# Late tiles of an attention and mixture-of-experts kernel placed by float32r products of two parts, and four of them in place of three

## The chip, the cores and the metric

One core of a Trainium2 chip. The metric is the device time of the whole kernel in microseconds; one profiled execution gives the trace, in which all rows below stand.

## The reference, cut to what matters

```python
y = decay_attention(r, k, v, w, u)            # batch 2, 8 heads, 768 steps, head size 48
x = y.transpose(0, 2, 1, 3).reshape(1536, 384)
expert = argmax(x @ w_gate, axis=1)           # 8 experts, one for each token
slot = number_of_earlier_tokens_of(expert)    # a token is dropped from slot 384 on
h = relu(rows_of_expert @ w1[e])              # 384 -> 1024
y = gate * (h @ w2[e])                        # 1024 -> 384, back in the tokens' order
out = (layernorm(solu(y @ w_in)) * g_ln) @ w_out
```

The attention runs over time in order, so the tokens of the last tiles are known last. An expert's product can only begin when the places of its tokens are known.

## The kernel before, in words

The 1536 tokens are 12 tiles of 128 rows. A first loop (`for t in range(NT)`, on every engine) computes one tile a step; step t also finishes tile t-1: TensorE splits the turned rows (`split_x`, L1515), VectorE takes the gate logits (`take_logits`, L1051), ScalarE copies the rows to SBUF (`take_x`, L784). For groups of tiles (`GROUPS`) VectorE picks the experts (`pick_experts`, L1057 to L1080) one step after the group's last tile, TensorE counts the earlier tokens (`count_before`, L1531 to L1536) two steps after it, and VectorE makes the slots (`place_tokens`, L1087 to L1095). GpSimd scatters the rows of each tile to their slots in a DRAM buffer that is sorted by expert (`scatter`, L556).

SP loads the rows of expert 0 as soon as the tiles ahead of `LATE` are scattered (L461 to L462). For each late tile VectorE makes a 0/1 matrix `columns_of` (`late_columns`, L1105 to L1115) that has a one where a token belongs to a row of expert 0, and TensorE multiplies the tile's rows by it (`place_late`, L1541 to L1547), accumulating in three PSUM banks; `place_first_rows` (L1549 to L1557) adds the rows that came from DRAM and raises `xe_turned` for each bank. ScalarE then takes the rounded part (`act_first_xe_hi`, L698 to L702) and VectorE the remainder (`dve_first_xe_lo`, L939 to L944), and the eight expert passes begin (`pe_up`, `pe_down`), each product there a pair of float32r products (L1357 with 448 columns, L1358 with 224). GpSimd scatters the late tiles for the other experts once SP's load of the first rows has landed (L624 to L627).

The order of work is written out by hand, and each engine runs its own list in order. On ScalarE a step is: `take_y` of the tile before (L771), the odd diagonal (`put_diagonal`, L758), `take_x`, `take_k` (L765), the even diagonal of the next step, `gate_exp` (L790), and in the last two steps one part of expert 0's first weights (`act_w1_hi`, L708). After the loop come `take_last_y` (L779), more weight parts, `take_x` of tile 11 and `act_w2_hi` (L714). On VectorE a step begins with two masks (`mask_scores`, L1034), of which the second waits for the odd diagonal; in each step stands `add_own` (L1016), whose result the diagonals need; after the loop come the last picks and columns, two remainders of weights (`lo_w1`, L512) and the remainders of the first rows. `columns_of` lies in the buffer of the scores, and the first column waits for the output of step 10 (L1114).

## Time and profile before

| | us |
|---|---|
| median of 3 runs | 330.14 (329.66 to 330.14) |
| the profiled execution | 329.34 |
| its span in the trace | 327.6 |
| TensorE busy | 312.2 (95% of the span) |
| VectorE, ScalarE, GpSimd busy | 210.9, 196.1, 187.8 |
| first product of pass 0 | starts at 81.37 |

The profiled execution is 1.7 us longer than its span and 0.8 us shorter than the median. Times in rows count from the start of the span. A row of a timeline gives the start, the length and, in brackets, how long the engine was idle before it and what ended that. An engine's next instruction may start before the one before has ended, so what an instruction takes of its engine is read from start to start. PE is TensorE, PEld its weight load; DVE is VectorE, ACT ScalarE, POOL GpSimd, and SPq the DMA queue of SP.

### The profile page before, as it was taken

To read this page: it belongs to the slowest core of one execution; us is meant where nothing else is said; L and a number is where in the kernel's file an instruction comes from. 1 tells how busy PE (TensorE), PEld (TensorE's weight loads), DVE (VectorE), ACT (ScalarE), POOL (GpSimd) and SP (SyncE) were. 2 spreads that over 40 slices of the span, in tenths; PEclk is the share of its full clock that TensorE was granted. 3 is DMA by queue.
4 is the path that set the end of the run, shared out by engine and by line. 5 is a ranking of instruction groups with operands and counts; after the bars stand their busy time and mean duration, and the time that the engine had idled before them with its cause. 6 is when DMAs were issued, how large, how long until landed. Compare 5 with 4: busy or idle time off the path is not lost.

```text
span 327.6 us, 6566 instructions
## 1 busy us (share of the span) xinstructions
PE 312.2 (95%) x2378; PEld 281.5 (86%) x2380; DVE 210.9 (64%) x479; ACT 196.1 (60%) x374; POOL 187.8 (57%) x170
## 2 busy tenths in 40 slices
PE   7799999988999999999999999999999999999991
PEld 3588888877999999999999999788999999999991
DVE  7757757797765746555555556888987676655610
ACT  2478776877666767667675757456565544543520
POOL 5966678971699797989898969401031111111221
PEclk9999999999999999999999999999999999999997
DMA  8999999893597948575666684000010000000010
GB/s 139 156 285 267 240 244 263 215 392 121 187 399 255 319 146 285 184 246 196 232 202 228 229 270 177 5 1 2 1 50 8 16 26 24 24 26 25 26 47 26
DMA packets 62898, 50.65 MB, mean 155 GB/s; under 512 B 42512, under 2 KB 58256, under 8 KB 62864
## 3 DMA queue, kind: packets, MB, share of 16 engines
q1 hardware_dynamic: 59104, 45.25, 47.7%
q0 software_dynamic: 1920, 4.73, 3.9%
q10 hardware_dynamic: 1840, 0.21, 0.9%
q8 instruction: 21, 0.34, 0.5%
q14 instruction: 13, 0.11, 0.1%
HBM read 38.37 MB, written 11.82 MB: 153 GB/s over the span
## 4 chain that ended last, share of the span: by engine, by line
PE 83%; POOL 4%; issue 4%; DVE 3%; DMA 3%; ACT 1%; DVEq 0%; POOLq 0%; ACTq 0%; SPq 0%
PE ps L1357 25%; PE ps L1648 15%; PE ps L1631 15%; PE ps L1358 12%; PE ps L1657 3%; PE ps L1515 2%; PE ps L1493 2%; PE ps L1461 2%; PE ps L1430 2%; DMA rk_in<-in_k_dram 2%; DMA u_all<-in_u_dram 1%; PE ps L1351 1%; POOL own_place L567 1%; POOL own_place L571 1%; PE ps L1476 1%
## 5 line engine op out<-in xcount | busy, mean ns | idle before, releaser
L512 POOL TENSOR_TENSOR w_lo<-w_raw,w_hi 128x768 fp32r<-128x768 f32 x33 | 60.4, 1855 | 10.3 <-DVE w_lo L518 9.8
L1357 PE MATMUL ps<-xe,w_hi 128*128 128x448 f32 x192 | 61.8, 378 | 0.3
L1357 PE MATMUL ps<-h,w_hi 128*128 128x448 f32 x192 | 61.8, 378 | 0.0
L1648 PE MATMUL ps<-w_hi,h 128*128 128x384 f32 x192 | 51.6, 340 | 0.0
L1358 PE MATMUL ps<-h,w_lo 128*128 128x224 f32 x192 | 50.9, 265 | 0.0
L1358 PE MATMUL ps<-xe,w_lo 128*128 128x224 f32 x192 | 50.8, 264 | 0.0
L664 POOL TENSOR_TENSOR rstd<-var_b,minus_half 128x1 f32<-128x1 f32 x12 | 6.8, 565 | 72.4 <-DVE var_b L1303 72.4
L1631 PE MATMUL ps<-w_hi,xe 128*128 128x512 f32 x144 | 46.5, 393 | 0.7 <-ACT xe L876 0.7
L949 DVE TENSOR_TENSOR ps<-ps,rk_in 128x448 f32<-128x448 f32 x32 | 20.2, 632 | 32.7 <-ACT rk_in L718 32.7
L1357 PEld LDWEIGHTS ps<-xe,w_hi 128*128 128x128 f32 x192 | 36.0, 188 | 4.9 <-issue 2.1
L518 POOL TENSOR_TENSOR w_lo<-w_raw,w_hi 128x1024 fp32r<-128x1024 f32 x16 | 38.1, 2406 | 1.9 <-DVE w_lo L518 1.9
L1357 PEld LDWEIGHTS ps<-h,w_hi 128*128 128x128 f32 x192 | 36.1, 188 | 2.7 <-ACT h L725 0.2
L1358 PEld LDWEIGHTS ps<-h,w_lo 128*128 128x128 f32 x192 | 36.7, 191 | 0.0
L1358 PEld LDWEIGHTS ps<-xe,w_lo 128*128 128x128 f32 x192 | 36.7, 191 | 0.0
L1648 PEld LDWEIGHTS ps<-w_hi,h 128*128 128x128 f32 x192 | 35.0, 188 | 0.0
L1631 PEld LDWEIGHTS ps<-w_hi,xe 128*128 128x128 f32 x144 | 27.1, 188 | 6.6 <-issue 1.2
L758 ACT ACTIVATE scores<-ident,own 128x128 f32<-128x128 f32 x92 | 29.3, 390 | 5.6 <-DVE own L1016 4.9
L1648 PE MATMUL ps<-w_lo,h 128*128 128x384 f32 x96 | 32.2, 336 | 0.0
L714 ACT ACTIVATE w_hi<-w_raw 128x1024 fp32r<-128x1024 f32 x24 | 24.5, 1055 | 8.6 <-PE ps L1358 7.9
L708 ACT ACTIVATE w_hi<-w_raw 128x768 fp32r<-128x768 f32 x36 | 29.4, 839 | 0.0
L1631 PE MATMUL ps<-w_lo,xe 128*128 128x512 f32 x72 | 28.2, 392 | 0.0
L1274 DVE TENSOR_REDUCE hmax<-ps 128x1 f32<-128x512 f32 x24 | 16.1, 686 | 18.2 <-PE ps L1631 18.2
(166 smaller groups left out, 617.3 us busy)
## 6 DMA issues: line engine op xcount, KB each, us to landing
w_raw<-in_moe_w_dram SPq DMA_DIRECT2D x15, 1536.0 KB, 7.4
x_slots<-zeros SPq DMA_DIRECT2D x6, 768.0 KB, 5.9
rk_in<-in_r_dram SPq DMA_DIRECT2D x12, 192.0 KB, 5.6
rk_in<-in_k_dram SPq DMA_DIRECT2D x12, 192.0 KB, 6.0
v_in<-in_v_dram SPq DMA_DIRECT2D x12, 192.0 KB, 5.5
out_dram<-zeros SPq DMA_DIRECT2D x1, 2304.0 KB, 8.1
w_raw<-in_moe_w_dram SPq DMA_DIRECT2D x3, 512.0 KB, 5.4
rows_in<-x_slots SPq DMA_DIRECT2D x8, 192.0 KB, 7.8
```

The source lines that it names most:

```text
L512: eng.tensor_tensor(w1_lo[:, :, cols], w1_raw[:, i, :, cols], w1_hi[:, :, cols].bitcast(F32), ALU.subtract).then_inc(g.w1_lo, 1)
L518: eng.tensor_tensor(w2_lo[:, :, cols], w2_raw[:, i, :, cols], w2_hi[:, :, cols].bitcast(F32), ALU.subtract).then_inc(g.w2_lo if d == 0 els ...
L708: act.activation(w1_hi[:, :, cols], w1_raw[:, i, :, cols], ACT.Copy).then_inc(hi_sem, 1)
L714: act.activation(w2_hi[:, :, cols], w2_raw[:, i, :, cols], ACT.Copy).then_inc(hi_sem, 1)
L758: last = act.activation(scores[:, t % 2, a, p, :], ident[:], ACT.Copy, scale=own[:, 2 * p + a:2 * p + a + 1])
L949: dve.tensor_tensor(first_sums(j, g.n), first_sums(j, g.n), h_rest[:, j % 2, :, 0:g.n], ALU.add)\
L1274: dve.tensor_reduce(hmax[:, a:a + 1], hidden_banks(t)[:, a, :], AX_X, ALU.max).then_inc(max_step, 1)
L1357: pe.matmul(ps[:, bank, 0:2 * n], w_hi, x[:, c, 0:2 * n], start=first, stop=False, skip_group_check=True)
L1358: return pe.matmul(ps[:, bank, 0:n], w_lo, x[:, c, 0:n], start=False, stop=last, skip_group_check=True)
L1631: last = pe.matmul(hidden_banks(t)[:, a, :], xt[:, c, i * P:(i + 1) * P], wt[:, c, a * 512:(a + 1) * 512], start=(c == 0 and z == 0), stop ...
L1648: last = pe.matmul(ps[:, OB + i, 0:DM], ht[:, f, i * P:(i + 1) * P], wt[:, f, :], start=(f == 0 and z == 0), stop=(f == KF - 1 and z == 2))
L1657: last = pe.transpose(ps[:, TB + f // 4, (f % 4) * P:(f % 4 + 1) * P], solu[i][:, f * P:(f + 1) * P], ident[:])
```

## The change

`LATE` gets a fourth tile, tile 8, and the group of tiles 6 to 8 becomes one of tiles 6 and 7 and one of tile 8 alone. For each late tile ScalarE writes the rows once more, rounded to float32r (`late_hi`), and GpSimd writes the remainder; TensorE places both by two float32r products where one float32 product stood. Both, and the columns, lie in the buffer `h` of the hidden layer, and the first column no longer waits for an output of the loop. The first late column is made within step 10, the last late tile is placed behind the first rows, and `xe_turned` is raised there. SP's load of the first rows waits for 8 scattered tiles in place of 9.

```diff
--- before.py
+++ after.py
@@ -143,8 +143,10 @@
 
 
 
-        LATE = [NT - 3, NT - 2, NT - 1]
-        columns_of = scores[:, 0].rearrange("p a h t -> p (a h t)")[:, 0:3 * N1].rearrange("p (t n) -> p t n", t=3)
+        LATE = [NT - 4, NT - 3, NT - 2, NT - 1]
+        h_place = h[:].rearrange("p f n -> p (f n)")
+        late_x = h_place[:, 0:2 * len(LATE) * DM].rearrange("p (t z d) -> p t z d", t=len(LATE), z=2)
+        columns_of = h_place[:, 2 * len(LATE) * DM:2 * len(LATE) * DM + len(LATE) * N1].rearrange("p (t n) -> p t n", t=len(LATE))
         column_key = rows_in[:, 1].rearrange("p m d -> p (m d)")[:, 0:N1]
         column_key_i = rows_in[:, 0].rearrange("p m d -> p (m d)")[:, 0:N1].bitcast(I32)
 
@@ -198,7 +200,7 @@
         EVEN_PAIRS = [h for h in range(H) if h // 2 % 2 == 0]
         ODD_PAIRS = [h for h in range(H) if h // 2 % 2 == 1]
         TOT = slice(CNT + 128, CNT + 128 + E)
-        GROUPS = [range(0, 3), range(3, 6), range(6, 9), range(9, 10), range(10, 11), range(11, 12)]
+        GROUPS = [range(0, 3), range(3, 6), range(6, 8), range(8, 9), range(9, 10), range(10, 11), range(11, 12)]
 
         HB, OB, TB = 0, 4, 6
         XA, XC = 2, 3
@@ -301,6 +303,8 @@
         first_odd_ready = sem("first_odd_ready")
         key_ready = sem("key_ready")
         columns_ready = sem("columns_ready")
+        late_x_hi = sem("late_x_hi")
+        late_x_lo = sem("late_x_lo")
         late_rank = sem("late_rank")
         late_slot_a = sem("late_slot_a")
         late_slot_b = sem("late_slot_b")
@@ -614,13 +618,17 @@
                             pool.wait_ge(picked_ready, n + 1)
                     own_parts(t + 1)
                 for _ in range(2):
-                    if t >= GROUPS[group_of(stored)][-1] + 4:
+                    if stored < LATE[0] and t >= GROUPS[group_of(stored)][-1] + 4:
                         if stored == 0:
                             pool.wait_ge(slots_zeroed, 16 * ZERO_PARTS)
                         scatter(stored)
                         stored += 1
             for t in range(stored, LATE[0]):
                 scatter(t)
+            for j in range(len(LATE)):
+                pool.wait_ge(late_x_hi, j + 1)
+                pool.tensor_tensor(late_x[:, j, 1], x_rows(LATE[j]), late_x[:, j, 0].bitcast(F32), ALU.subtract)\
+                    .then_inc(late_x_lo, 1)
             for m in range(usual.tiles):
                 pool.wait_ge(usual.rows_loaded[0][m], 16)
             for t in LATE:
@@ -784,6 +792,10 @@
                 act.activation(x_rows(t).rearrange("p (q n) -> p q n", q=HP), pairs_of_x()[:, :, 0:2 * D], ACT.Copy)\
                     .then_inc(x_ready, 1)
 
+            def late_hi(j):
+                act.wait_ge(x_ready, LATE[j] + 1)
+                act.activation(late_x[:, j, 0], x_rows(LATE[j]), ACT.Copy).then_inc(late_x_hi, 1)
+
             def gate_exp(n):
                 g = GROUPS[n]
                 act.wait_ge(below_ready, n + 1)
@@ -806,12 +818,15 @@
                 for n, g in enumerate(GROUPS):
                     if t == g[-1] + 2:
                         gate_exp(n)
+                if t - 1 in LATE:
+                    late_hi(LATE.index(t - 1))
                 if t >= NT - 2:
                     act_w1_hi(act, 0, usual.w1_in[0], w1_loads(0, 1), usual.w1_hi, parts=[t - NT + 2])
             take_last_y()
             gate_exp(len(GROUPS) - 2)
             act_w1_hi(act, 0, usual.w1_in[0], w1_loads(0, 1), usual.w1_hi, parts=[2])
             take_x(NT - 1)
+            late_hi(len(LATE) - 1)
             act_w1_hi(act, 0, usual.w1_in[0], w1_loads(0, 1), usual.w1_hi, parts=[3])
             gate_exp(len(GROUPS) - 1)
             act_w2_hi(act, 0, usual.w2_in[0], 16, usual.w2_hi, parts=[0, 1])
@@ -1111,7 +1126,6 @@
                 dve.wait_ge(late_slot_a, j + 1)
                 if j == 0:
                     dve.wait_ge(key_ready, 2)
-                    dve.wait_ge(y_done, NT - 1)
                 dve.tensor_scalar(columns_of[:, j], column_key, slot_a[:, t:t + 1], None, ALU.is_equal).then_inc(columns_ready, 1)
 
             def late_slots():
@@ -1156,14 +1170,16 @@
                         else:
                             place_tokens(n)
                         add_picked(n)
-            late_columns(0)
-            rank_late(1)
+                        if g[-1] == LATE[0]:
+                            late_columns(0)
+            late_columns(1)
+            rank_late(2)
             add_picked(len(GROUPS) - 2)
             take_logits(NT - 1)
             pick_experts(len(GROUPS) - 1)
-            late_columns(1)
-            rank_late(2)
             late_columns(2)
+            rank_late(3)
+            late_columns(3)
             late_slots()
             add_picked(len(GROUPS) - 1)
 
@@ -1541,10 +1557,13 @@
             def place_late(j):
 
                 pe.wait_ge(columns_ready, j + 1)
-                pe.wait_ge(x_ready, LATE[j] + 1)
+                pe.wait_ge(late_x_lo, j + 1)
                 for c in range(KD):
-                    pe.matmul(first_turned(c), x_rows(LATE[j])[:, c * P:(c + 1) * P], columns_of[:, j],
-                              start=(j == 0), stop=False, skip_group_check=True)
+                    for z in range(2):
+                        last = pe.matmul(first_turned(c), late_x[:, j, z, c * P:(c + 1) * P], columns_of[:, j],
+                                         start=(j == 0 and z == 0), stop=(j == len(LATE) - 1 and z == 1), skip_group_check=True)
+                    if j == len(LATE) - 1:
+                        last.then_inc(usual.xe_turned, 1)
 
             def place_first_rows():
 
@@ -1552,9 +1571,8 @@
                     pe.wait_ge(usual.rows_loaded[0][m], 16)
                 for c in range(KD):
                     for m, rows in enumerate(usual.rows):
-                        last = pe.matmul(first_turned(c)[:, m * P:m * P + rows], rows_in[0:rows, 0, m, c * P:(c + 1) * P],
-                                         ident[0:rows, 0:rows], start=False, stop=(m == 1), skip_group_check=True)
-                    last.then_inc(usual.xe_turned, 1)
+                        pe.matmul(first_turned(c)[:, m * P:m * P + rows], rows_in[0:rows, 0, m, c * P:(c + 1) * P],
+                                  ident[0:rows, 0:rows], start=False, stop=False, skip_group_check=True)
 
             pe.wait_ge(zero_ready, 1)
             keep_warm(10, UB)
@@ -1583,10 +1601,11 @@
             count_before(len(GROUPS) - 2)
             split_x(NT - 1)
             place_late(0)
+            place_late(1)
             count_before(len(GROUPS) - 1)
-            place_late(1)
             place_late(2)
             place_first_rows()
+            place_late(3)
             pe.wait_ge(sum_ready, len(GROUPS))
             pe.wait_ge(late_rank, len(LATE))
             pe.matmul(ps[:, UB, TOT], ones_bf[:], picked_sum[:], start=True, stop=True).then_inc(total_done, 1)
```

## Rows read from the trace of the kernel before

**Rows 1.** Windows: us; busy us (x instructions) per engine; granted clock; DMA share; GB/s
```profile
68.44:75.19 6.75, 5.18 (x70) 4.45 (x69) 5.93 (x26) 5.87 (x17) 3.59 (x5) 1.00 1.02 407
75.19:81.37 6.18, 5.61 (x35) 4.84 (x35) 4.90 (x19) 4.04 (x9) 0.97 (x1) 1.00 0.20 70
...
81.37:210.00 128.63, 127.85 (x814) 119.66 (x815) 76.61 (x130) 85.48 (x136) 111.93 (x63) 1.00 0.65 226
```

**Rows 2.** Chain of waits: start us, us, what; around the last late tiles
```profile
74.22 1.15 PE ps L1515 x8
...
76.74 0.35 DVE scores L1115
...
77.13 2.54 PE ps L1546 x12
...
79.75 1.55 PE ps L1555 x12
```

**Rows 3.** Timeline of ScalarE, step 9 to the first rows: start us, us, instruction
```profile
63.68 0.57 ACT L771 ACTIVATE yt<-ps 128x512 f32<-128x512 f32 x1
...
66.63 0.49 ACT L784 ACTIVATE w_raw<-ps 128x384 f32<-128x384 f32 x1 [1.20 <-DVE logits L1051]
67.01 0.59 ACT L765 ACTIVATE place<-ps 128x512 f32<-128x512 f32 x1
...
69.11 0.21 ACT L790 ACTIVATE lexp<-below 128x24 f32<-128x24 f32 x1
69.22 0.83 ACT L708 ACTIVATE w_hi<-w_raw 128x768 fp32r<-128x768 f32 x1
69.96 0.57 ACT L771 ACTIVATE yt<-ps 128x512 f32<-128x512 f32 x1
...
72.58 0.49 ACT L784 ACTIVATE w_raw<-ps 128x384 f32<-128x384 f32 x1 [0.88 <-DVE logits L1051]
...
80.44 1.25 ACT L702 ACTIVATE xe<-ps 128x224 fp32r<-128x224 f32 x3 [1.61 <-PE ps L1555]
```

**Rows 4.** Timeline of TensorE: the splits of tiles 9 and 10
```profile
64.72 1.14 PE L1515 MATMUL ps<-pick_pair,yt 128*128 128x104 f32 x8
...
70.58 1.14 PE L1515 MATMUL ps<-pick_pair,yt 128*128 128x104 f32 x8 [0.98 <-ACT yt L771]
```

**Rows 5.** Timeline of TensorE: neighbouring float32r products in pass 0
```profile
84.74 0.26 PE L1358 MATMUL ps<-xe,w_lo 128*128 128x224 f32 x1
84.84 0.38 PE L1357 MATMUL ps<-xe,w_hi 128*128 128x448 f32 x1
85.05 0.26 PE L1358 MATMUL ps<-xe,w_lo 128*128 128x224 f32 x1
```

**Rows 6.** Timeline of VectorE: outliers, weight remainders, remainders of the first rows
```profile
63.23 1.50 DVE L1080 TENSOR_TENSOR picked<-lscore,top 128x24 bf16<-128x24 f32 x1
...
68.55 0.60 DVE L1095 SCALAR_TENSOR_TENSOR slot<-slot_a,slot_b 128x3 int32<-128x3 f32 x1
...
78.37 1.82 DVE L512 TENSOR_TENSOR w_lo<-w_raw,w_hi 128x768 fp32r<-128x768 f32 x2
80.83 1.29 DVE L943 TENSOR_TENSOR xe<-ps,xe 128x224 fp32r<-128x224 f32 x3 [0.64 <-ACT xe L702]
```

**Rows 7.** GpSimd: costliest groups on the page, then its timeline
```profile
L512 POOL TENSOR_TENSOR w_lo<-w_raw,w_hi 128x768 fp32r<-128x768 f32 x33 | 60.4, 1855 | 10.3 <-DVE w_lo L518 9.8
...
72.01 0.97 POOL L556 DMA_INDIRECT x_slots<-w_raw,slot  x1 [0.30 <-issue]
80.38 0.97 POOL L556 DMA_INDIRECT x_slots<-w_raw,slot  x1 [7.40 <-DMA rows_in<-x_slots]
```

**Rows 8.** SP's queue, then DMA issues with us to landing
```profile
77.08 0.81 SPq L457 DMA_DIRECT2D rows_in<-x_slots  x2
...
rows_in<-x_slots SPq DMA_DIRECT2D x1, 192.0 KB, 2.2
...
meta<-token,sorted_to POOLq DMA_INDIRECT x12, 6.4
```

## The prediction

> **What bounds the kernel now.** I read the stages first [rows 1]. From 81.37 us on, TensorE is busy 127.85 of 128.63 us: the expert passes are bound by TensorE, and the change edits nothing in them. So it can only move the moment at which the first product of pass 0 starts, 81.37 us, and everything behind that moment keeps its distance to it. Ahead of it lie two stretches in which TensorE is not full: 68.44 to 75.19 (5.18 busy of 6.75) and 75.19 to 81.37 (5.61 of 6.18), all at a granted clock of 1.00, the 2.4 GHz level.
>
> The chain of waits says what those two stretches hang on [rows 2]: the split of the last chunk on TensorE (L1515, 74.22), the last tile's logits and picks on VectorE, the column of a late tile (L1115, 76.74), then two placements (L1546, 77.13, 2.54 us) and the first rows (L1555, 79.75, 1.55 us). Last I read the engines' own timelines, because ScalarE stands ahead of this chain: its rows from 69.11 to 69.96 are back to back [rows 3], and before the split of tile 10 TensorE sat idle 0.98 us for ScalarE's L771 [rows 4].
>
> **The change, part by part.**
>
> *Placement on TensorE.* Before, a late tile is three float32 products; the trace records two MATMULs for each, so 12 records are two tiles: 2.54 / 2 = 1.27 us a tile [rows 2]. After, it is six float32r products of 224 columns, each with its own weight load. The nearest row is a float32r product of the same 224 columns, L1358: 84.74 to the start of its successor at 84.84, 0.10 us [rows 5]. There a 448-column neighbour may cover the load, so the upper bound is the product of the first rows, the narrowest with a load of its own: 1.55 / 12 = 0.129 us [rows 2]. I take 0.11: 0.66 us a tile (bounds 0.60 and 0.77), 0.61 less than now. The Trainium skill ("TensorE: Matmul & The Clock Gate", LDWEIGHTS) gives a load as columns / 1.2, 107 ns for 128; by that estimate a tile is 0.64 us, the two results being 0.02 us apart.
>
> Four tiles cost 4 x 0.66 = 2.64 against 3.81 us, but two of the four (8 and 9) go ahead of the last count, where TensorE waits for picks anyway. On the path stood 2.54 (two tiles) + 1.55, with the first `xe_turned` after a third of the rows: 2.54 + 0.08 + 0.52 = 3.14 us after 77.13, and ScalarE's L702 starts at 80.44 [rows 3]. After, it is one tile, all rows, and a third of the last tile: 0.66 + 1.55 + 0.22 = 2.43. Gain at `xe_turned`: 0.7 us.
>
> *What that gain runs into.* VectorE must first end the two weight remainders that start at 78.37 and last 1.82 us (to 80.19), and its L943 then sat idle 0.64 us [rows 6]. These precede the remainders of the first rows in VectorE's order and stay there. So of the 0.7 us at most 0.64 can be had; ScalarE was idle 1.61 us before L702 and takes tile 11's new copy within that.
>
> *ScalarE's four new copies* (`late_hi`, 128x384, SBUF to float32r). The nearest row is L784, the same 384 elements: 66.63 to the next start at 67.01, 0.38 us of the engine [rows 3]; L708 with 768 elements goes 69.22 to 69.96, 0.74, so half of it is 0.37 and no less. One more group also adds a `gate_exp`, 69.11 to 69.22, 0.11. Three copies stand in the loop, each *ahead of* the next `take_y` and `put_diagonal`:
> - Step 9: `gate_exp` and tile 8's copy push `take_y(9)` from 63.68 to 64.17. TensorE's split of tile 9 starts at 64.72 and needs it at 64.17 + 0.57 = 64.74: no loss. The split's row is in [rows 4]. But the odd diagonal, the second mask, the logits and `take_x(9)` (66.63) all go 0.49 later. The diagonal after it also waits for VectorE's `own`, which depends on GpSimd and moves less; I take 0.11 as regained (bounds 0 and 0.49). Shift 0.38.
> - Step 10: tile 9's copy stands ahead of `act_w1_hi` part 0 and `take_y(10)`: 69.96 becomes 70.72. Shift 0.76. This is the wait that shows as 0.98 us before L1515; it grows. The odd diagonal comes right behind it, and the mask that waits for that diagonal and the logits follow.
> - Step 11: `take_x(10)` (72.58), then tile 10's copy, then part 1 of the weights, then L779. Shift 1.14.
>
> So the split of tile 11 starts at 74.22 + 1.14 = 75.36, and the picks, columns and weight remainders on VectorE behind it go 1.14 later too. The Trainium skill ("ScalarE: Activation LUTs", What ACT_TABLE_LOAD costs) gives an ACTIVATE with immediates 186 ns + 0.833 ns an element and 93 ns of overlap back to back: an estimate of 0.41 us a copy, which makes the shift 1.14 + 3 x 0.03 = 1.23. Its 506 ns for one agrees with the 0.49 us of the row; the overlap is what differs.
>
> The trace's 0.38 stands in my sum.
>
> *VectorE.* Step 8 gains the pick of tiles 6 and 7; step 9 gets their placing, an `add_picked` and one single-tile pick in place of a pick of three tiles, some ten operations of about 0.2 us where five were; step 10 loses about as much and gains a column. That delays the first mask of step 10, but the second one waits for the odd diagonal anyway; cost 0, and up to 1.3 us if an outlier like the 1.50 us L1080 at 63.23 or the 0.60 us L1095 at 68.55 falls there, where the copies of such size take about 0.2 [rows 6]. After the loop its work is what it was: the fourth column is made within step 10.
>
> *GpSimd.* Four subtractions of 128x384, half of L512's 1.855 us for 768 elements each, 0.93 us [rows 7]. They stand between the early scatters and a wait that was 7.40 us long. The fourth waits for tile 11's copy, which ends some 2.3 us after the split that starts at 75.36 (split 1.15, logits 0.2, `take_x` and copy 0.49 each), near 77.7, and so ends near 78.6; its product is due about 80.5. Cost 0. Behind them in its queue stand the late scatters, four instead of three, each 0.97 + 0.30 us: from 79.7 they end near 84.8, and a weight part of 1.86 us after them ends at 86.7. Its product is the 19th pair of pass 0, which at 0.31 us a pair (84.74 to 85.05 [rows 5]) comes near 87.5. Cost 0, with 0.8 us of cover. SP's loads for pass 1 wait for these scatters too and go out some 0.8 us later; they are wanted a whole pass on. Cost 0.
>
> *SP's load of the first rows.* It waits for the scatters ahead of the late tiles: 9 before, 8 after. The last one started at 72.01 [rows 7] and the load was issued at 77.08, 5.07 us later, landing 2.2 us after issue [rows 8]. Tile 7's scatter starts one scatter (1.27) and the old wait for slots (0.3) earlier, near 70.4: by 5.07, loads at 75.5, both landed at 75.5 + 0.43 + 2.2 = 78.1. Wanted: 77.13 + 1.14 + 0.66 = 78.93. Cost 0; cover 0.8 us.
>
> *Sum.* By TensorE: 77.13 + 1.14 + 2.43 = 80.70 for `xe_turned`, against 80.27; ScalarE + 0.43. By VectorE: 80.19 + 1.14 = 81.33 for its first remainder, against 80.83: + 0.50. VectorE ends last, so pass 0 starts at 81.87 and the span is 0.50 us longer. The profiled execution, 329.34 us, becomes 329.84. The median of the runs shown is 330.14, 0.8 above the profiled one, so for the median I give 330.14 + 0.5 = 330.6. A measurement of this kernel can tell about 0.2% (0.66 us) from no change: 0.5 us is within it.
>
> **Rivals.**
> 1. *The first rows come late* (slower). Tile 7's scatter lies wholly in the stretch where the DMA engines are full (407 GB/s, against 70 behind 75.19) [rows 1], tile 8's had the drained end; the scatters of tokens landed after 6.4 us [rows 8]. By 6.4 us the loads go out at 76.8, land at 79.4, 0.5 us too late, and the products of rows and of the last tile stand behind them in TensorE's order: + 0.95 us, 331.1. It decides from a landing over 78.9 on. If the scatter gains nothing at all and rows land at 79.7, + 1.3, 331.4. Against it: a head start of 1.3 us or more. Chance 0.2.
> 2. *ScalarE's idle time takes the copies.* It was idle 1.20 and 0.88 us before its two L784 in the trace [rows 3]. If the copies of tiles 8 and 9 vanish there, the shift is 0.38 and VectorE's 0.64 of idle outweighs it: -0.26, 329.9; with none left, -0.64, 329.5. Against it: each copy stands behind the wait, not in it, ahead of work that the next step wants. Chance 0.15.
> 3. *VectorE becomes the bound in steps 9 and 10*, by stretched small operations of the new group: + 0.5 to + 1.3 beyond my sum, 331.1 to 331.9. For it: 63.23 and 68.55. Chance 0.1.
> 4. *The placement is not cheaper* (0.21 us for each product, as each record of L1546 takes now): a tile stays at 1.27 us, the path is 1.27 + 1.55 + 0.42 = 3.24 against 3.14, and with the shift pass 0 starts 1.24 us later, 331.4. The 0.10 us of L1358 speaks against it. Chance 0.03.
>
> **How the numbers follow.** My own case, shift of 0.9 to 1.3 us and VectorE last, gives + 0.3 to + 0.7, 330.4 to 330.8: chance 0.5; it reaches 0.2% only at its top. 0.02 is left for what I don't see. The range takes rival 2 to its -0.64 and rivals 1 and 3 up to + 1.5: 329.5 to 331.7. Faster by over 0.2% needs more than the whole 0.64 of VectorE's idle time: 0.07. Slower by over 0.2%: rivals 1, 3 and 4 (0.33) and a little of my own case: 0.38. Within: 0.55.
>
> **What would show it.** Right: L1546 at about 0.11 us a record; ScalarE's copies of 0.49 us directly ahead of L771; the wait before the split of tile 10 grown from 0.98 to about 1.4 us; the last split at 75.3; no idle time on VectorE before L943; pass 0 starting at 81.9; the stages behind it unchanged. Wrong: TensorE idle before the first rows with a DMA as releaser (rival 1); the last split still at 74.3 (rival 2); a late mask in step 10 or 11 with VectorE busy before it (rival 3). A change of the passes' own length would overturn the frame.

## The result and the profile after

The kernel after takes 332.75 us (median of 20 executions, 330.43 to 334.78), the kernel before, beside it, 329.61 us (20 executions, 328.35 to 330.41): a ratio of 1.008 [1.0061, 1.01], so the change makes it slower by 0.8%. The profiled execution of after took 331.01 us with a span of 329.2: 1.67 us more than the profiled execution of before. The prediction, 330.6 us and no measurable difference as the likeliest case, was wrong, and 332.75 lies above its range.

Two things have to be explained: the 1.67 us that the profiled executions differ by, and why the median of 20 executions lies another 1.7 us above the profiled one. For the first, the windows of after: step 10 of the loop, and then the stretches of [rows 1], cut at the same events (the columns are those of [rows 1]):

```profile
63.44:69.58 6.14, 5.92 (x84) 4.99 (x82) 5.96 (x17) 4.49 (x14) 5.75 (x7) 1.00 1.01 350
69.58:76.95 7.37, 5.13 (x70) 4.39 (x69) 6.00 (x23) 6.49 (x18) 5.20 (x6) 1.00 0.82 326
76.95:83.21 6.26, 4.97 (x43) 4.42 (x42) 5.65 (x19) 4.81 (x11) 2.34 (x3) 1.00 0.17 58
83.21:211.84 128.63, 127.77 (x816) 119.50 (x816) 76.80 (x130) 85.28 (x135) 112.78 (x64) 1.00 0.66 228
```

The expert passes are what they were, 128.63 us in both, and what follows them is 0.2 us shorter. Pass 0 starts at 83.21 in place of 81.37, 1.84 us later, and all of it arises ahead of it. TensorE's timeline says where:

```profile
63.44 1.71 PE L1477 MATMUL ps<-place 64*128 64x128 f32 x16
65.69 1.14 PE L1531 MATMUL ps<-pick_pair,yt 128*128 128x104 f32 x8
...
69.58 1.16 PE L1477 MATMUL ps<-place 64*128 64x128 f32 x16
71.94 1.14 PE L1531 MATMUL ps<-pick_pair,yt 128*128 128x104 f32 x8 [1.19 <-ACT yt L779]
...
76.04 1.14 PE L1531 MATMUL ps<-pick_pair,yt 128*128 128x104 f32 x8 [0.60 <-ACT yt L787]
76.95 1.58 PE L1563 MATMUL ps<-h 128*128 128x224 f32 x12
...
79.75 0.93 PE L1563 MATMUL ps<-h 128*128 128x224 f32 x6 [0.98 <-DVE h L1129]
80.52 1.48 PE L1574 MATMUL ps<-ident,rows_in 128*128 128x128 f32 x12
81.78 0.91 PE L1563 MATMUL ps<-h 128*128 128x224 f32 x6
...
83.21 0.44 PE L1373 MATMUL ps<-xe,w_hi 128*128 128x448 f32 x1 [0.27 <-ACT xe L710]
```

The first product of a step (L1477; L1461 before) and the splits (L1531; L1515 before) can be laid beside those of before:

| start, us | step 10 | step 11 | split of tile 10 | split of tile 11 | pass 0 |
|---|---|---|---|---|---|
| before | 63.01 | 68.44 | 70.58 | 74.22 | 81.37 |
| after | 63.44 | 69.58 | 71.94 | 76.04 | 83.21 |
| later by | 0.43 | 1.14 | 1.36 | 1.82 | 1.84 |

Of the 0.43 us, 0.38 is there at step 8 already (52.85 against 52.47), where no edited instruction has run; the runs below start their step 8 between 52.47 and 53.84, so this much is an offset of the execution. (The three latest, 53.56 to 53.84 in `a1_same`, `g2_all` and `f2_three_warm`, are the traces in which the granted clock was 0.50 from about 16 to 19 us, far ahead of anything that was edited; all others start it at 52.91 or sooner.) The change itself costs 1.46 us: 0.05 in step 9, 0.71 in step 10 (6.14 us long against 5.43), 0.68 from the start of step 11 to the last split, and 0.02 behind it, where 0.64 us was to be won.

ScalarE, the copies (L797) and what stands behind them (beside [rows 3]):

```profile
70.16 0.51 ACT L797 ACTIVATE h<-w_raw 128x384 fp32r<-128x384 f32 x1
70.57 0.83 ACT L716 ACTIVATE w_hi<-w_raw 128x768 fp32r<-128x768 f32 x1
71.31 0.58 ACT L779 ACTIVATE yt<-ps 128x512 f32<-128x512 f32 x1
...
74.46 0.52 ACT L797 ACTIVATE h<-w_raw 128x384 fp32r<-128x384 f32 x1
74.89 0.83 ACT L716 ACTIVATE w_hi<-w_raw 128x768 fp32r<-128x768 f32 x1
75.62 0.64 ACT L787 ACTIVATE yt<-ps 128x256 f32<-128x256 f32 x2
```

A copy takes 0.41 and 0.43 us of ScalarE from start to start (0.38 was expected; tile 11's, from 77.96 to 78.40, takes 0.44), and the two splits wait 1.19 us in place of 0.98 and 0.60 in place of 0.15 for exactly the work behind it.

GpSimd and VectorE are the surprise (beside [rows 6, 7]). First GpSimd, then VectorE:

```profile
64.19 1.02 POOL L583 TENSOR_TENSOR place<-rk_in,wlast 128x384 f32<-128x384 f32 x1
...
75.06 0.99 POOL L630 TENSOR_TENSOR h<-w_raw,h 128x384 fp32r<-128x384 f32 x1 [0.80 <-ACT h L797]
78.57 1.00 POOL L630 TENSOR_TENSOR h<-w_raw,h 128x384 fp32r<-128x384 f32 x1 [2.51 <-ACT h L797]
```

```profile
63.70 1.55 DVE L1076 SCALAR_TENSOR_TENSOR lscore<-logits,lmax,desc 128x8 f32<-128x8 f32 x1
...
65.48 0.34 DVE L1081 TENSOR_SCALAR picked<-lscore,top 128x8 bf16<-128x8 f32 x1
...
65.87 1.52 DVE L1049 COPY_PREDICATED scores<-causal,ps 128x512 f32<-128x512 int32 x2
...
75.22 0.97 DVE L1129 TENSOR_SCALAR h<-rows_in,slot_a 128x224 fp32r<-128x224 f32 x1
...
78.56 1.14 DVE L1129 TENSOR_SCALAR h<-rows_in,slot_a 128x224 fp32r<-128x224 f32 x1
...
80.01 0.34 DVE L1129 TENSOR_SCALAR h<-rows_in,slot_a 128x224 fp32r<-128x224 f32 x1
...
80.88 1.81 DVE L516 TENSOR_TENSOR w_lo<-w_raw,w_hi 128x768 fp32r<-128x768 f32 x2
82.67 0.99 DVE L958 TENSOR_TENSOR xe<-ps,xe 128x224 fp32r<-128x224 f32 x3
```

The same column (L1129) takes 0.34 us with GpSimd idle and 0.97 and 1.14 us beside a remainder on GpSimd. Each long one ends with the GpSimd instruction: 78.56 + 1.14 = 79.70 against 78.57 + 1.00 = 79.57; 75.22 + 0.97 = 76.19 against 76.05; and 63.70 + 1.55 = 65.25 against 64.19 + 1.02 = 65.21. I call this a hold. The masks (L1049, one operand from PSUM) aren't held: two take 1.52 us beside GpSimd and took as much before. The outliers of [rows 6] are holds too: 63.23 + 1.50 = 64.73, while a GpSimd product ran from 63.66 to 64.68. The Trainium skill ("SBUF — State Buffer", SBUF: two separate sides) names a port pair that VectorE and GpSimd share as an exclusive lock, taken by whichever starts first, among others where a VectorE instruction has two SBUF inputs and the GpSimd one reads SBUF. The lengths agree with it, even for an instruction of 128x8 elements. Who goes first can't be read from the recorded starts: VectorE's is the earlier one, by 0.01 us at 78.56, by 0.49 at 63.70 and by 0.43 in the row of before at 63.23, and yet VectorE was held.

The wait of 0.98 us at 79.75 is such a hold. Last, TensorE's timeline prices the placement: from 79.75 to 80.52 a tile takes 0.77 us, not 0.66.

### The profile page after: what moved, and what is told of

It reads as the page before. It is cut to its first block, busy times and chain, and to the rows that moved or that the text cites. A ratio compares the mean times of both kernels' runs of the same rounds, so it can differ in the third digit from the quotient of the medians.

```text
span 329.2 us, 6608 instructions
## 1 busy us (share of the span) xinstructions
PE 312.5 (95%) x2387; PEld 281.7 (86%) x2387; DVE 214.6 (65%) x489; ACT 198.1 (60%) x379; POOL 192.3 (58%) x174
## 4 chain that ended last, share of the span: by engine, by line
PE 86%; ACT 4%; DVE 3%; issue 2%; POOL 1%; DMA 1%; DVEq 0%; SPq 0%; POOLq 0%; ACTq 0%
PE ps L1373 25%; PE ps L1667 15%; PE ps L1650 15%; PE ps L1374 12%; PE ps L1509 4%; PE ps L1676 3%; PE ps L1531 3%; PE ps L1477 3%; PE ps L1446 2%; ACT scores L766 2%; PE ps L1504 1%; PE ps L1492 1%; PE ps L1367 1%; DMA wsq<-in_w_dram 1%; DVE place L977 1%
```

## The experiments

Twelve runs in three groups, each group with runs of the kernel before on the same chip: 31 executions with a median of 330.58 us for the a-kernels; 25, 329.91 us, for b, c and f1; 33, 330.2 us, for g, f2 and h1. Each group stands under its texts of expectation, which name theories: **L**, VectorE's instructions are held by GpSimd's remainders; **C**, ScalarE's copies ahead of `take_y` cost; **D**, the pick of the new group's tile 8 delays step 10; **G**, idle time lets TensorE's granted clock fall in some executions; **N**, nothing but noise.

### The change again, the copies and the holds

`a1_same` is the kernel after, unchanged.

> The changed kernel once more, unchanged, beside the others. Its 20 executions lie in two heaps, near 331.1 and near 333.5 us, and the granted clock of a whole execution is 0.99 in most of the first and 0.98 in most of the second. Theory G (TensorE's clock falls to its lower level in some executions): such an execution shows a stretch with a granted clock below 1.00 after one of the waits ahead of pass 0, and is 2 to 3 us longer. Theory N (only noise in the loads): the clock is 1.00 everywhere up to the end and the spread comes from the loop. Both expect a ratio of 1.006 to 1.010.

332.04 us, ratio 1.0048 [1.0022, 1.0075]. Slower again, by less. Its trace has the same holds of the columns (0.97 and 1.14 us) and a last split 6.32 us into step 11 (6.46 in after), but its step 10 takes 5.73 us where that of after took 6.14, with the same code: a single trace can be off by 0.4 us there. Between 50 and 90 us its granted clock is 1.00, so this trace shows nothing for theory G; two of the 12 executions have a mean clock under 0.988.

`a2_waits` lets each GpSimd remainder wait until VectorE's columns are made:

```diff
                 pool.wait_ge(late_x_hi, j + 1)
+                pool.wait_ge(columns_ready, [1, 2, 2, 4][j])
```

> GpSimd's remainder of tile 8 waits for the first column, those of tiles 9 and 10 for the second, that of tile 11 for the fourth, so that no column is written while a remainder runs. Theory L (VectorE's column from two SBUF operands is held while GpSimd's remainder runs): L1129 takes 0.34 us each of the last three times instead of 0.97, 1.14 and 0.34, the third column is ready 0.8 us earlier, and pass 0 starts 0.7 to 0.8 us earlier than in the changed kernel; 0.7 us off the time in the faster heap. Theory C alone (only the copies on ScalarE cost): the columns keep their lengths, no gain.

332.19 us, 1.0041 [1.0019, 1.0064]. The holds of the columns are gone and nothing is won. VectorE's timeline says why:

```profile
78.43 0.34 DVE L1130 TENSOR_SCALAR h<-rows_in,slot_a 128x224 fp32r<-128x224 f32 x1
...
79.87 0.98 DVE L1136 SCALAR_TENSOR_TENSOR slot<-slot_a,slot_b 128x4 int32<-128x4 f32 x1
...
81.01 1.81 DVE L516 TENSOR_TENSOR w_lo<-w_raw,w_hi 128x768 fp32r<-128x768 f32 x2
```

The last remainder now runs from 79.83 to 80.83 and holds the slots: 0.98 us where 0.16 is usual. TensorE is done with its last tile at 81.7, 0.8 us earlier than in after, and then waits 1.38 us for VectorE, whose weight remainders start at 81.01 against 80.88. A hold that is moved is still a hold, and behind the last column VectorE is the one that counts.

`a3_later` takes the copies out from ahead of `take_y` (tile 10's stands before the last `take_x`); `a4_both` is this and the wait of `a2_waits`:

```diff
             put_diagonal(t, 1)
+                if t - 2 in LATE:
+                    late_hi(LATE.index(t - 2))
...
-                if t - 1 in LATE:
-                    late_hi(LATE.index(t - 1))
...
+            late_hi(len(LATE) - 2)
```

> The copies of tiles 8, 9 and 10 go on ScalarE behind the odd diagonal of the next step, ahead of a wait for the logits of 0.9 to 1.2 us, tile 10's ahead of the last take_x. Theory C (they cost because they stand ahead of take_y): the last split of TensorE starts 1.1 us earlier than in the changed kernel, pass 0 starts 0.5 to 1.1 us earlier. Theory L alone: the remainders of GpSimd start later and still meet the columns, gain below 0.3 us. Theory G: if the wait before the split of tile 10 is what lets the clock fall, the slower heap is gone and the median falls by over 2 us.

> Both edits together. Theories C and L together: pass 0 starts 1.5 to 1.9 us earlier than in the changed kernel, at about 81.3, and the time is that of the kernel before or up to 0.6 us less (ratio 0.998 to 1.001). If one of the two is wrong, half of it.

332.96 us, 1.0056 [1.0028, 1.0083], and 332.03 us, 1.0043 [1.002, 1.0067]. From the start of step 11 to the last split takes 5.73 and 5.45 us, against 6.46 in after and 5.78 before: C holds, the copies cost those 0.68 us. But pass 0 starts at 83.69 and 83.16, where about 81.3 was expected of `a4_both`. Of the 83.69, 0.7 us are lost in steps 8 and 9, which take 5.53 and 5.74 us in this trace (5.27 and 5.32 in after), though the edit leaves step 8 alone and takes a copy out of step 9. The rest is in VectorE's timeline of `a3_later`:

```profile
77.61 0.87 DVE L1077 SCALAR_TENSOR_TENSOR lscore<-logits,lmax,desc 128x8 f32<-128x8 f32 x1
...
78.70 0.85 DVE L1082 TENSOR_SCALAR picked<-lscore,top 128x8 bf16<-128x8 f32 x1
```

Two remainders of GpSimd (77.43 to 79.53) now meet the last pick and hold two of its instructions, 0.64 and 0.62 us over the 0.23 us that each takes otherwise. In `a4_both` VectorE's weight remainders are the end, as in `a2_waits`: the last pick (0.98 us at 76.80) and the slots (0.98 us at 79.76) are held there. The four ratios of this group can't be told apart; what each edit does is read from the traces.

### The parts alone

`c1_nolo` has no remainders on GpSimd. It leaves that part of the computation out: TensorE multiplies the rounded part twice, so its work stays the same.

```diff
-            for j in range(len(LATE)):
-                pool.wait_ge(late_x_hi, j + 1)
-                pool.tensor_tensor(late_x[:, j, 1], x_rows(LATE[j]), late_x[:, j, 0].bitcast(F32), ALU.subtract)\
-                    .then_inc(late_x_lo, 1)
```

> GpSimd's four remainders are left out (a part of the computation: each late row goes in by its rounded part twice, so TensorE's work is the same). Theory L (GpSimd's remainders hold VectorE's operations on two or one SBUF operands): the second and third column take 0.34 us each instead of 0.97 and 1.14, VectorE starts its last two weight remainders 0.9 us earlier, and pass 0 starts 0.8 to 1.0 us earlier than in the changed kernel; what stays against the kernel before is about 0.5 to 1.0 us. Theory C alone: less than 0.2 us off.

331.04 us, 1.0038 [1.0015, 1.006]. The columns behind the loop:

```profile
74.85 0.34 DVE L1125 TENSOR_SCALAR h<-rows_in,slot_a 128x224 fp32r<-128x224 f32 x1
...
78.86 0.34 DVE L1125 TENSOR_SCALAR h<-rows_in,slot_a 128x224 fp32r<-128x224 f32 x1
```

Both take 0.34 us, and so does the last. The column of step 10, at 68.95 beside GpSimd's products of the keys, is held as in after (0.80 us; 0.73 there). L is shown: take the GpSimd instruction away and the hold goes. Pass 0 starts at 82.76, 0.45 us earlier than in after, where 0.8 to 1.0 was expected. The trace says what took the difference; first its windows, then TensorE's timeline:

```profile
72.00:74.00 2.00, 1.73 (x29) 1.50 (x29) 1.37 (x8) 1.12 (x5) 0.07 (x1) 0.92 1.02 397
74.00:76.00 2.00, 2.00 (x19) 1.63 (x16) 1.21 (x8) 1.99 (x7) 0.00 (x0) 0.50 0.26 101
```

```profile
71.59 1.14 PE L1527 MATMUL ps<-pick_pair,yt 128*128 128x104 f32 x8 [1.19 <-ACT yt L775]
...
75.68 1.80 PE L1527 MATMUL ps<-pick_pair,yt 128*128 128x104 f32 x8
```

The granted clock is 0.50, the 1.2 GHz level, from about 74 to 77 us, 2 us behind a wait of 1.19 us, the very wait that after has before its split of tile 10. The last split takes 1.57 us to the next start in place of 0.91, which is 0.66 us; with the 0.45 that makes 1.1 us, an estimate of what the kernel without remainders gains at an unchanged clock. Against the kernel before, some 0.7 us are left without any remainder.

`b2_nosplit` keeps the new groups and the four late tiles, but places them by the old float32 product: no copies, no remainders, the columns in a buffer of their own (`late_columns_place`).

```diff
-                    for z in range(2):
-                        last = pe.matmul(first_turned(c), late_x[:, j, z, c * P:(c + 1) * P], columns_of[:, j],
-                                         start=(j == 0 and z == 0), stop=(j == len(LATE) - 1 and z == 1), skip_group_check=True)
+                    last = pe.matmul(first_turned(c), x_rows(LATE[j])[:, c * P:(c + 1) * P], late_columns_place[:, j],
+                                     start=(j == 0), stop=(j == len(LATE) - 1), skip_group_check=True)
```

> The fourth late tile and the new groups alone, with one float32 product for each as before (no copies, no remainders). Theory D: the steps from the start of step 10 to that of step 11 take 5.9 to 6.3 us as in the changed kernel, against 5.43 before. Theories C and L alone: 5.5 us, and the last split starts no later than before by more than 0.2 us. Two float32 tiles of 1.27 us stand ahead of the last count, so pass 0 starts 1.0 to 1.5 us later than before whichever holds: ratio 1.003 to 1.006.

330.66 us, 1.0021 [1.0006, 1.0035], below the 1.003 to 1.006 that was expected, though pass 0 starts at 82.63, 1.26 us later than before, as expected. Step 10 takes 5.95 us against 5.43 before, with no copy in the kernel: this is D. All traces together bear it out: step 10 takes 5.73 to 6.30 us in the eight with the new group picked behind the placing (after, `a1_same` to `a4_both`, `b2_nosplit`, `c1_nolo`, `f1_warm`), and 5.36 to 5.68 in the four with the old groups (before, `b1_three`, `f2_three_warm`, `h1_best`). What happens can be read in the rows of after above. In both kernels an instruction of the pick is held until GpSimd's product of the keys ends, 1.67 us after the start of step 10 before and 1.77 us in after. Before, the held one was the last of the pick (L1080, [rows 6]), and the masks started at 64.65 (start to start an overlap of 0.08 us). After, placing tiles 6 and 7 stands ahead of the pick, the held one is its second (L1076), and L1079 to L1083 follow, so the masks start at 65.87: 2.43 us into the step, against 1.64. Their results feed the new state (L1062), and TensorE's count waits for that. Behind the loop the split of tile 11 starts 5.57 us into step 11, 0.21 less than before.

`b1_three` is the split alone: three late tiles and the old groups, with copies and remainders.

```diff
-        LATE = [NT - 4, NT - 3, NT - 2, NT - 1]
+        LATE = [NT - 3, NT - 2, NT - 1]
-        GROUPS = [range(0, 3), range(3, 6), range(6, 8), range(8, 9), range(9, 10), range(10, 11), range(11, 12)]
+        GROUPS = [range(0, 3), range(3, 6), range(6, 9), range(9, 10), range(10, 11), range(11, 12)]
```

> The split alone: three late tiles and the groups of before. Theory C+L: the last split of TensorE starts 0.8 us later than before (two copies in the loop), columns and picks are held by the remainders of tiles 10 and 11, ratio to before 1.002 to 1.004, and no loss in step 9 to 10. Theory D (the new group in step 9 is what costs): ratio within 1.000 to 1.001.

333.16 us, 1.0099 [1.0068, 1.0129] of 6 executions, where 1.002 to 1.004 was expected: worse than the whole change. Step 10 is back at 5.47 us, which bears out D from the other side. What it lost is in the windows and TensorE's timeline:

```profile
77.00:78.00 1.00, 0.33 (x3) 0.14 (x2) 0.89 (x6) 0.97 (x3) 0.00 (x0) 1.00 0.00 0
78.00:79.00 1.00, 0.19 (x2) 0.13 (x2) 0.97 (x1) 1.00 (x3) 0.97 (x1) 0.84 0.86 277
79.00:85.00 6.00, 5.79 (x27) 5.61 (x28) 3.70 (x12) 2.68 (x6) 3.11 (x4) 0.50 0.20 80
85.00:86.00 1.00, 1.00 (x6) 0.94 (x6) 0.90 (x6) 1.00 (x2) 0.00 (x0) 0.74 0.48 197
```

```profile
78.05 0.17 PE L1545 MATMUL ps<-picked,tri_bf 128*128 128x8 bf16 x1 [0.72 <-DVE picked L1081]
...
79.22 1.62 PE L1561 MATMUL ps<-h 128*128 128x224 f32 x6 [0.97 <-DVE h L1129]
80.64 2.74 PE L1572 MATMUL ps<-ident,rows_in 128*128 128x128 f32 x12
83.08 1.60 PE L1561 MATMUL ps<-h 128*128 128x224 f32 x6
```

From 79 to 85 us the granted clock is 0.50, the 1.2 GHz level, and the products of the first rows take 2.74 us in place of 1.48. In the two windows ahead of it TensorE was busy 0.33 and 0.19 of 1 us, in the second because its column (78.03, 1.13 us) was held. The Trainium skill ("TensorE: Matmul & The Clock Gate", What's actually happening) describes a clock that falls after idle time of the engine; the trace agrees in kind, and what stands ahead of the fall are waits of 1.26, 0.72 and 0.97 us with work between them.

This can be seen in the times of all executions, since each has its mean granted clock. Six us at half clock lower the mean over 330 us by 6 x 0.5 / 330 = 0.009, from about 0.993 to 0.984. The executions with a mean under 0.988:

| kernel | under 0.988 | kernel | under 0.988 |
|---|---|---|---|
| before, 89 beside the runs below | 3 | c1_nolo | 1 of 12 |
| after | 7 of 20 | b2_nosplit | 0 of 12 |
| a1_same | 2 of 12 | g1_pickfirst | 2 of 10 |
| a2_waits | 1 of 10 | g2_all | 3 of 12 |
| a3_later | 5 of 10 | h1_best | 1 of 12 |
| a4_both | 1 of 12 | f1_warm | 0 of 8 |
| b1_three | 5 of 6 | f2_three_warm | 0 of 12 |

The count is a lower bound and a rough one: the stretch of 3 us in `c1_nolo` leaves a mean of 0.991, and the early one at 16 us, which has nothing to do with the change, leaves 0.990 in `a1_same` and 0.989 in `f2_three_warm`. Nor is a low mean always a long time: the five of `a3_later` have a median of 332.58 us, the other five 332.96.

The 7 of after have a median of 333.56 us, the other 13 of 331.35, which is 1.74 above before's 329.61, as in the traces (1.67).

`f1_warm` puts products of zeros (`keep_warm`, about 0.25 us each) where TensorE of after waits: four ahead of the split of tile 10, two ahead of the last, four ahead of the tile that waits for the held column.

```diff
+                if t == NT - 1:
+                    keep_warm(4, RT)
...
+            keep_warm(2, RT)
...
+                keep_warm(4, RT)
             place_late(2)
```

> The changed kernel with ten products of zeros for TensorE in its three waits of 1.19, 0.60 and 0.98 us (4, 2 and 4 of some 0.22 us each). Theory G (executions with a mean clock below 0.988 are the ones in which TensorE's idle time lets the clock fall): none below 0.988, against 7 of 20 and 2 of 12 of the changed kernel and none of 31 of the kernel before, and no execution above 333 us on this chip's scale. If the clock falls for another reason the share stays near a quarter. The best executions are not faster than without (0 to +0.2 us).

331.21 us, 1.0036 [1.0018, 1.0055]. None of its 8 executions is under 0.988. Pass 0 starts at 82.87, as far behind step 8 as in after (30.40 us against 30.36).

### Repairs

`g1_pickfirst` picks tile 8 ahead of the placing of tiles 6 and 7.

```diff
+                if t == LATE[0] + 1:
+                    pick_experts(group_of(LATE[0]))
...
-                    if t == g[-1] + 1:
+                    if t == g[-1] + 1 and g[-1] != LATE[0]:
```

> The changed kernel, with tile 8 picked ahead of the placing of tiles 6 and 7 in step 9, so that the pick no longer meets GpSimd's product for the next keys. Theory D (the pick of the new group is held there for 1.3 us and delays step 10): the 1.5 us operation in step 9 is gone, the start of step 10 to that of step 11 takes 5.4 to 5.6 us instead of 6.14, pass 0 starts 0.5 us earlier than in the changed kernel. If the stall has another cause (TensorE itself paused in step 10 of the changed kernel), it stays at 5.9 or more.

331.55 us, 1.0052 [1.0034, 1.007]. The 1.5 us instruction is gone. Step 10 takes 5.70 us (5.4 to 5.6 was expected) against 6.14 in after; but `a1_same`, which doesn't have this edit, shows 5.73, so what the order is worth isn't shown by this run. The wait before the split of tile 10 grew, 1.50 against 1.19 us, since it hangs on ScalarE, and pass 0 starts at 83.27, where about 82.7 was expected.

`g2_all` adds to this the copies moved as in `a3_later` (tile 10's right behind `take_last_y`) and the remainders on VectorE:

```diff
-                pool.tensor_tensor(late_x[:, j, 1], x_rows(LATE[j]), late_x[:, j, 0].bitcast(F32), ALU.subtract)\
+                dve.tensor_tensor(late_x[:, j, 1], x_rows(LATE[j]), late_x[:, j, 0].bitcast(F32), ALU.subtract)\
```

> All three causes taken away from the changed kernel: the pick order of g1, ScalarE's copies in its idle time (tile 10's right behind the last take_y), and the remainders on VectorE (tile 8's in step 11, 9's and 10's before the last logits, 11's behind the last column) instead of GpSimd. Theories C, L and D together: no held operation above 0.5 us beside the two first steps, pass 0 starts at 81.4 to 82.0, ratio 0.999 to 1.002. If one of them is wrong, ratio 1.003 or more.

331.54 us, 1.005 [1.003, 1.007], where 0.999 to 1.002 was expected. Step 10 takes 5.30 us, less than before. Its profiled execution has a mean clock of 0.978 (the early stretch at 16 us is in it too) and shows the fall once more, in its windows, 2 us behind a wait of 1.35 us that ended at 71.97:

```profile
73.00:74.00 1.00, 0.74 (x19) 0.47 (x17) 1.00 (x3) 0.50 (x2) 0.00 (x0) 0.92 1.05 407
74.00:80.00 6.00, 5.68 (x35) 5.38 (x36) 4.62 (x25) 4.66 (x11) 0.00 (x0) 0.50 0.31 111
```

The clock doesn't account for the miss: its nine executions that aren't under 0.988 have a median of 331.31 us, still 1.1 above before. Taking L, C and D away doesn't repair the kernel with four late tiles. In its trace the remainders, 0.5 us each, now stand on VectorE's own path: one ahead of the second mask of step 11, for which TensorE waits 0.59 us (0.27 in after), and one behind the last column, so that the weight remainders start 6.49 us behind the last split (4.84 in after) and TensorE waits 1.34 us for VectorE before pass 0. Some of these 6.49 us are the lower clock; how much isn't shown.

`f2_three_warm` is `b1_three` with the products of zeros: four ahead of the split of tile 10, two ahead of the last count of the loop, two ahead of the last split, five ahead of the tile of the held column.

```diff
+                if t == NT - 1:
+                    keep_warm(4, RT)
...
+            keep_warm(2, RT)
...
+            keep_warm(2, RT)
+            keep_warm(5, RT)
```

> b1_three (three late tiles, split; five of its six executions had a mean clock below 0.988 and its trace a stretch at 0.50 from 79 to 85 us) with 13 products of zeros in TensorE's waits. Theory G: no execution below 0.988, the time 2.0 to 2.5 us less than b1's 333.2, ratio 1.002 to 1.004. If the lower clock is not from the idle time, the ratio stays near 1.010.

331.6 us, 1.0043 [1.0023, 1.0063], against 1.0099 [1.0068, 1.0129] without them: the intervals don't meet, and none of 12 executions is under 0.988 where 5 of 6 were. Nothing else in the kernel differs; the two ran on different chips, each with the kernel before beside it. G is shown for this kernel, and it is worth about 0.56% there. The holds and copies are still in it, and with them the other 0.4%.

`h1_best` takes the causes away rather than their effects: three late tiles and the old groups, the copies in ScalarE's waits, the remainders on VectorE, one weight remainder of VectorE's behind those of the first rows, and one load of weights on SP behind the load of the first rows. As a diff to `b1_three`, shortened:

```diff
-            load_w1(1, 1)
...
+            load_w1(1, 1)
...
+            late_lo(0)
+            late_lo(1)
...
+            late_lo(2)
...
-            lo_w1(dve, 0, 0, usual, parts=[1, 2])
+            lo_w1(dve, 0, 0, usual, parts=[1])
...
+            lo_w1(dve, 0, 0, usual, parts=[2])
```

> A version that might beat both: the groups and three late tiles of before, placed by split products; copies on ScalarE in its idle time, remainders on VectorE, VectorE's third weight remainder moved behind the first rows' remainders, and SP's load of expert 1's first weights (1536 KB) issued behind the load of the first rows so that the scatters land earlier. If theories C, L and D are right and nothing else binds: the last split as early as before, the first rows loaded before 77, pass 0 starts 0.6 to 1.0 us earlier than before, ratio 0.996 to 0.999. If the scatters' landing does not depend on that load, the first rows still come at 79.7 and the ratio is 1.000.

329.93 us against 330.2, 0.9993 [0.9972, 1.0015]: as fast as before, not faster. TensorE's timeline:

```profile
77.96 0.93 PE L1567 MATMUL ps<-h 128*128 128x224 f32 x6 [0.17 <-DVE h L1126]
78.72 1.48 PE L1578 MATMUL ps<-ident,rows_in 128*128 128x128 f32 x12
79.99 0.91 PE L1567 MATMUL ps<-h 128*128 128x224 f32 x6
...
81.41 0.44 PE L1377 MATMUL ps<-xe,w_hi 128*128 128x448 f32 x1 [0.49 <-ACT xe L706]
```

The last split starts at 74.92, 5.55 us into step 11 (6.46 in after), no column is held, and pass 0 starts at 81.41 against 81.37; counted from step 8 (52.83 and 52.47) that is 0.32 us earlier, where 0.6 to 1.0 was expected. SP's load of the first rows is issued at 75.23, 2.54 us behind the start of the scatter that it waits for (72.69), against 5.07 us before: from 70 to 72 us the busy share of the DMA engines is 0.18, where it is 1.03 in before with the load of weights still under way. The run makes several edits at once, and what each is worth isn't shown. No version that ran beats the kernel before by more than can be measured.

## Why the prediction was wrong

**What the prediction got right.** The expert passes didn't change. ScalarE's copies shift the last split, though by luck the size looks better than it is: 1.14 us were predicted for them, and the split moved by 1.44 (the offset of 0.38 taken off), but only the 0.68 us of step 11 are theirs. In step 9 next to nothing was lost (0.05 us), and of the 0.71 us of step 10 VectorE's part is 0.5, by `b2_nosplit`. The wait before the split of tile 10 grew (1.4 predicted, 1.19 measured). VectorE has no idle time before the remainders of the first rows, so its 0.64 us were used up as said. SP's load of the first rows was not the bound, though the reason given was wrong: it was issued at 77.10, as before (77.08, [rows 8]), and not at 75.5, though the scatter that it waits for started at 71.30, 0.7 us earlier. This is the second case of rival 1, rows at 79.7 (77.10 + 0.43 + 2.2), and `h1_best` speaks for its reason, the full DMA engines. TensorE reached the rows 1.6 us later than was reckoned, at 80.52 against 78.93, and that hid it: luck, and not a cover of 0.8 us.

**The step that failed: "GpSimd. [...] Cost 0".** The prediction counted when GpSimd would be done and who waits for its results. It didn't ask what VectorE can do while GpSimd works. The last remainder (1.00 us long, 0.93 reckoned) held the third column for 0.80 us (1.14 against 0.34), on the path of both engines: TensorE waited 0.98 us for that column, and VectorE's weight remainders start 2.51 us later than before (80.88 against 78.37), of which 1.82 are the late split and 0.69 came behind it. Evidence: the ends of the rows coincide, `c1_nolo` removes it, `a2_waits` and `a3_later` move it onto other instructions of VectorE.

**"VectorE. [...] cost 0, and up to 1.3 us if an outlier [...] falls there"** is the same error seen from the other side. The 1.50 us at 63.23 was no outlier: a GpSimd product ended 0.05 us before it. The sum had seen that the new group delays the first mask and let the second one's wait for the odd diagonal hide it. In the trace both masks ran one behind the other with no wait, 0.79 us late in the step, and the count of step 10 waited for what they feed. That is rival 3 with its mechanism, and 0.5 us of step 10's 0.71 by `b2_nosplit` (5.95 against 5.43). Rival 3 reached up to 331.9 in the prediction's own words, and the range, which ended at 331.7, cut it off.

**The sum, put right.** Predicted: 1.14 - 0.64 = +0.50 us. Measured in the profiled execution, by VectorE: offset 0.38, shift 1.44, hold 0.69, less 0.64 of VectorE's idle time: 1.87 us. By TensorE and ScalarE: offset 0.38, shift 1.44, hold 0.80, less the 0.78 us by which the way from the placement behind the column to pass 0 is shorter (79.75 to 83.21 against 77.13 to 81.37): 1.84 us, and pass 0 does start 1.84 us later, with ScalarE as the one it waited for. So both ways end within 0.03 us of each other, and taking the hold off one of them alone, as in `a2_waits`, wins nothing.

**Mis-sized terms.** The placement takes 0.77 us a tile, the upper bound that was given, not 0.66: L1358 with 0.10 us stands between products of 448 columns, which may cover its load (no run takes that apart), and the product of the first rows with its own load (1.55 / 12) was the right row. A copy takes 0.41 to 0.44 us of ScalarE, not 0.38.

**The second step that failed: the clock, priced at nothing without a reason.** The windows of before showed 1.00 in every stage that was read, and I took this for granted. The prediction said that waits would grow, 0.98 to 1.4 us, and priced only the wait itself. In 7 of 20 executions of after the mean clock is lower by about what 6 us at 0.50 make, and these are 2.2 us longer at the median; this moves the median of all from 331.35 to 332.75. It is 1.4 of the 2.64 us by which the change exceeded the predicted 0.50.

**What stays open.** The kernel after gave 1.008 at first and 1.0048 [1.0022, 1.0075] when repeated; the intervals overlap, and how often the clock falls (7 of 20, then 2 of 12) is the difference that I can name. It doesn't explain everything: three executions of after took over 333.3 us at a mean clock of 0.989 to 0.997, and in `a3_later` the executions with the low mean aren't the long ones. In step 10, after shows 1.71 us for L1477 where 1.16 is usual. This pause is there in `a1_same` to `a4_both` too, with 0.2 to 0.4 us, but not in `b2_nosplit`, `c1_nolo` and `f1_warm`, whose step 10 is as long within 0.2 us because the count waits for VectorE there (0.48 us in `b2_nosplit`, 0.55 in `f1_warm`); its cause I don't know. That the clock fell because of the idle time is shown for `b1_three` by `f2_three_warm`; for after it is inferred, from `c1_nolo`, whose clock fell behind the same wait of 1.19 us in TensorE's same order of work, since `f1_warm`'s 0 of 8 against `a1_same`'s 2 of 12 settles nothing and no execution of after with a low mean was profiled. What keeps four late tiles slower than before in `g2_all`, with L, C and D taken away, is open too; `h1_best` with four late tiles wasn't tried.

## What to carry to other kernels

Work put on a "free" GpSimd is not free while VectorE is on the path: before it is costed at nothing, lay its interval over VectorE's, and read a VectorE instruction that takes several times its usual length, and ends with one of GpSimd's, as a hold. Moving the GpSimd instruction only chooses who is held, so give it to an engine that is idle or to a stretch in which VectorE reads PSUM or waits; on VectorE itself it takes that engine's time, as in `g2_all`. Where a change makes TensorE wait longer in an already thin stretch, look at the clock in every execution and not in one trace.

## What the runs showed of the hardware that was not expected

- A VectorE instruction of 8 elements a partition takes 0.23 us alone and, beside GpSimd's products of the keys, 1.55 us in after and 1.79 us in `a3_later`; it ends 0.04 us behind the last of them, and the columns 0.13 and 0.14 us behind the remainder. A mask from PSUM and the reductions ran at their usual length beside GpSimd.
- The granted clock fell to 0.50 for 6 us in `b1_three` behind two stretches of 1 us with 0.33 and 0.19 us of work, in `g2_all` 2 us behind a wait of 1.35 us, and for 3 us in `c1_nolo` 2 us behind a wait of 1.19 us. With products of zeros in such waits none of 20 executions had a mean under 0.988, both traces are at 1.00 from 50 to 86 us, and pass 0 of `f1_warm` starts no later for them.
- Two float32r products that each bring their load take 0.77 / 3 = 0.26 us together, one float32 product of the same 224 columns 2.54 / 6 = 0.42 us: a tile is cheaper by 0.5 us on TensorE, and the copy that it needs costs 0.4 us on ScalarE.
- From the start of the last early scatter to the load that waits for it, 5.07 us passed in before, with the DMA engines at a busy share of 1.03 from 70 to 72 us, and 2.54 us in `h1_best`, with 0.18.
